# Mixed tiles of two experts in place of padded tiles, and a reordered convolution step, in a two-layer mixture of experts

## The chip, the cores and the metric

One core of a Trainium2 chip runs the program. The metric is the device time of one execution in microseconds; the median of three runs of the kernel before is 1354.1 (1354.05 to 1354.81). TensorE (PE) multiplies, VectorE (DVE) and ScalarE (ACT) work on tiles, GpSimd (POOL) issues the scatters, SyncE (SP) issues most of the other transfers. All times below are microseconds unless marked ns.

## What is computed

A causal convolution of seven taps over the sequence, with softmax taps for each head, and then two mixture-of-experts layers with one expert for each token. N is 14336 tokens of 192 values, 8 experts, 1024 hidden values. Cut to what matters:

```python
x = attn_out.reshape(N, 192)                # causal convolution, 7 taps for each of 8 heads
for layer in (0, 1):
    logits = x @ w_gate
    expert_idx = np.argmax(logits, axis=1)
    gate_w = softmax(logits)[np.arange(N), expert_idx]
    for e in range(8):
        mask = expert_idx == e
        h = np.maximum(x[mask] @ w1[e], 0.0)
        out[mask] = gate_w[mask, None] * (h @ w2[e])   # layer 1: times sigmoid(x @ w_output_gate)[mask, e] too
    x = out
```

## The kernel before

**Convolution steps.** Eight steps (`STEPS`) of 16 windows of 112 tokens. In each, PE convolves, DVE finds the largest value of each row and its power of two (`largest`), ACT and DVE scale the rows and split them into two float16 parts (`hi_ready`, then `low_rows`, lines 1029 and 1030), PE transposes them and computes the logits, DVE chooses an expert and a place (`step_choose`, `step_place`), and POOL writes the rows with 16 indirect DMAs (line 531) into the DRAM tensor `rows[0]`, in which each expert has a region of `CAP` rows. Beside it each step turns the weights of one expert of layer 0 into scaled float16 parts: SP loads them into `stage` (lines 332 to 337), DVE reduces them (`weights_max`, lines 1090 and 1092), POOL takes the maximum over partitions (`weight_maxima`, line 525), DVE makes the scale (`weights_scale`), ACT writes the high part and DVE the low part (`weights_lo`, lines 1105 and 1108), and SP stores the image and loads the next `stage` of that slot.

**Tables.** From the number of rows of each expert DVE makes a table (`table_counts`, `table_tiles`, `table_scales`): for each tile its first row and its expert. An expert with c rows gets ceil(c/256) tiles. Whatever the counts are, N/256 + E - 1 = 63 tiles a layer (`NT`) are enough, and 63 are always run; the last one or more can be empty. Rows behind the last row of an expert are filled by `store_pad` (line 350) with pad rows. In layer 1 the first 11 tiles (`EARLY`) are listed before the last rows of layer 0 are placed, and the rest later. The list is dealt out to even and odd tiles, so that each of the two weight slots keeps its expert over several tiles.

**Expert tiles.** A tile is 256 rows of one expert. `hidden` multiplies in four chunks (`NP`), each a PSUM bank of 2 x 256 columns: for each half of a chunk four matmuls of 256 columns, and `hidden_low` adds eight matmuls of 64 rows, which run in pairs in the two halves of the array. ACT takes the relu and its float16 high part (`relu_hi`, line 732), DVE the low part (`hidden_lo`, line 1214), and `contract` multiplies back, with 12 matmuls of 192 columns a chunk. `contract` of tile t for chunks 1 to 3 runs between the hidden chunks of tile t+1. In layer 0 the finished rows of each two tiles (a pair) are split, transposed, gated and scattered into `rows[1]`; tiles 4 to 35 of layer 0 also prepare the weights of layer 1.

**SP's queue in a tile** (`loads`, line 406): it waits until the hidden chunks of the tile before are done (`h_done`), reads from the table in SBUF the experts of tile g+1 and of tile g-1 (`expert`), which had the same slot, loads part 0 of the image (1 MB) only if they differ (line 404), and otherwise raises the semaphore itself; then `load_x` of tile g+2: one table read, two DMA transposes (lines 395 and 396) and the load of two values of each row (line 397); then it waits for `y_done` and does part 1 of the weights. `xT` has four buffers (`XS`), `wslot` has two.

What sets the order: each engine's queue is written out in program order, with semaphores between them; the first four tiles (`HEAD`), tiles 60 to 67 around the change of layer (`MID`) and the last (`TAIL`) are unrolled, the others are loops of four tiles.

Of the kernel before, what the change touches and what calls it, by code (L numbers as in the profile page):

```python
# [18 lines left out]
B, S, D = 4, 3584, 192  # L19
H, K = 8, 7  # L20
E, F = 8, 1024
N = B * S
P = 128
# [20 lines left out]
NT = N // T + E - 1  # L44
GT = 2 * NT
EARLY = 11
STAGES = ((0, 0, NT), (1, NT, EARLY), (1, NT + EARLY, NT - EARLY))
QUADS = NT // 4
PAIRS = (NT + 1) // 2
# [23 lines left out]
def build(nc, x, weight, wg0, w10, w20, wg1, wo1, w11, w21, out):  # L73
# [12 lines left out]
    with ctx:  # L86
# [10 lines left out]
        onesf = sb("onesf", [1, 1], f32)  # L97
# [8 lines left out]
        tidx = sb("tidx", [P, GT], f32)  # L106
# [58 lines left out]
        took = sb("took", [P, E], f32)  # L165
        start = sb("start", [P, 1], f32)
        ge = sb("ge", [P, NT, E], f32)
        gt = sb("gt", [P, NT, E], f32)
        te = sb("te", [P, NT], f32)
        tst = sb("tst", [P, NT], f32)  # L170
        tew = sb("tew", [P, NT], f32)
        tabD = sb("tabD", [P, GT], f32)
        tab = sb("tab", [P, 2, GT], i32)
# [65 lines left out]
        routed = sem("routed")  # L239
        token_ready = sem("token_ready")  # L240

        w_loaded = [[sem(f"w{part + 1}_loaded{i}") for i in range(2)] for part in range(2)]
        x_loaded = [sem(f"x_loaded{i}") for i in range(XS)]
        meta_loaded = [sem(f"meta_loaded{i}") for i in range(XS)]
        meta_out = sem("meta_out")
# [7 lines left out]
        FIRST = (NT // 2 + 1, NT // 2)  # L253
# [37 lines left out]

        def routes(g, s, l):
# [11 lines left out]
        HEAD, MID = range(0, 4), range(4 * QUADS, 4 * QUADS + 8)  # L304
        LOOPS = (((1, E + 1, True), (E + 1, QUADS, False)), ((QUADS + 2, GT // 4, False),))
        TAIL = range(GT // 4 * 4, GT)
        LAST = (GT - 1, (GT - 1) // 2, 1)
        assert NT % 4 == 3 and E + 1 < QUADS and STEPS == E and SPB == 2
# [14 lines left out]

        def pair_wins(p):

            return J if isinstance(p, int) and p == PAIRS - 1 else W2T
# [27 lines left out]
        def _(sp):  # L354
# [36 lines left out]

            def load_x(g, x, l):
                r0 = sp.value_load(tab[0:1, 1, bass.ds(g, 1)], min_val=0, max_val=ROWS - T)
                tile_rows = rows[l][bass.ds(r0, T), :]
                sp.dma_start_transpose(xT[:, x, 0:3, :], tile_rows.bitcast(f16)[:, 0:3 * P]).then_inc(x_loaded[x], 16)  # L395
                sp.dma_start_transpose(xT[:, x, 3:4, :], tile_rows.bitcast(f16)[:, DB:DB + P]).then_inc(x_loaded[x], 16)
                sp.dma_start(xmeta[:, x, :, :], tile_rows[:, D:RW].rearrange("(j p) c -> p j c", j=J)).then_inc(meta_loaded[x], 16)

            def expert(g):
                return sp.value_load(tab[0:1, 0, bass.ds(g, 1)], min_val=0, max_val=E - 1)  # L400

            def load_w_part(e, l, s, part):
                cols = (slice(0, W2H), slice(W2H, WCOL))[part]
                sp.dma_start(wslot[:, s, cols], images[l][bass.ds(e + l, 1), :, cols].rearrange("e p c -> (e p) c")).then_inc(w_loaded[part][s], 16)

            def loads(g, k, s, v, i, prep, l):
# [3 lines left out]
                ahead = layer_of(g + 1, l)  # L410

                def load_next(e, had, part):
                    if other:
                        load_w_part(e, ahead, 1 - s, part)
                    else:
                        with sp.If(e != had):
                            load_w_part(e, ahead, 1 - s, part)
                        with sp.Else():
                            sp.sem_inc(w_loaded[part][1 - s], 16)
# [20 lines left out]
            for e in range(E // 2):  # L440
                store_pad(sp, 0, e)
# [933 lines left out]
```

## Time and profile before

| | |
|---|---|
| median of 3 runs | 1354.1 us (1354.05 to 1354.81) |
| profiled execution | 1355.4 us, span 1353.8 us |
| instructions | 38270 |
| busy share | PE 90%, DVE 64%, ACT 47%, POOL 33% |
| mean granted clock of TensorE | 0.929 |
| tiles | 63 in each of two layers |

The page gives for each engine its busy time and share of the span, and the span in 40 slices of 33.8 us. The timeline gives single instructions with start and duration; in brackets stands how long the engine sat idle before an instruction and what released it. SPq is SP's queue: the duration of a DMA instruction there is the time for which it occupies the queue, not that of the transfer.

### The profile page before, as it was taken

What the parts mean: (1) busy time and instruction counts of PE and PEld (TensorE: products, weight loads), DVE (VectorE), ACT (ScalarE), POOL (GpSimd) and SP (SyncE); (2) the same over time, 40 slices, a digit from 0 to 9 for tenths busy, and PEclk for the clock granted to TensorE, in tenths of its full rate; (3) what the DMA queues carried; (4) which work ended last, traced back from release to release, by engine and by line L of the source; (5) the groups of instructions that cost most, each with busy time, mean ns of one, the idle gap of its engine ahead of it and who ended that gap; (6) DMA issues with size and microseconds to landing.
All of it is one profiled execution on the core that took longest, in us unless ns stands there. A gap on an engine that the chain in (4) does not pass through costs nothing.

```text
span 1353.8 us, 38270 instructions
## 1 busy us (share of the span) xinstructions
PE 1214.6 (90%) x13162; PEld 1092.6 (81%) x13162; DVE 869.7 (64%) x2322; ACT 638.7 (47%) x1126; POOL 451.5 (33%) x480
## 2 busy tenths in 40 slices
PE   3777683099999999999999999999999999999998
PEld 2666673088888888889999998888899999899997
DVE  3798887348999999997777777633433334333333
ACT  2676674135555555654444544433333333333342
POOL 1187777503333443332222222422222222222222
PEclk9666665599999999999999999999999999999999
DMA  8388856646876677553522246356442244262220
GB/s 231 90 261 272 254 191 193 212 99 160 228 191 159 160 195 206 140 150 84 130 50 55 54 102 147 74 148 166 109 110 61 56 103 106 57 164 59 55 52 17
DMA packets 237528, 181.20 MB, mean 134 GB/s; under 512 B 183263, under 2 KB 215675, under 8 KB 233890
## 3 DMA queue, kind: packets, MB, share of 16 engines
q1 hardware_dynamic: 209760, 114.76, 34.5%
q0 software_dynamic: 26096, 64.50, 15.6%
q10 hardware_dynamic: 1618, 1.26, 0.3%
q8 instruction: 29, 0.48, 0.2%
q14 instruction: 25, 0.20, 0.1%
HBM read 79.36 MB, written 70.80 MB: 111 GB/s over the span
## 4 chain that ended last, share of the span: by engine, by line
PE 56%; DVE 20%; issue 9%; DMA 7%; SPq 5%; ACT 2%; POOL 1%; DVEq 1%; ACTq 0%; POOLq 0%
PE bank L791 55%; DMA stage<-in_moe_w 5%; DVE hl L1214 2%; DVE wam L1090 2%; DVE split L1105 2%; DVE am L1021 1%; PE bank L796 1%; DVE xsl L1025 1%; DVE split L1108 1%; ACT rowt L642 1%; DMA wslot<-image 1%; POOL rows L531 1%; DVE rowab L1030 1%; DVE rowt L1030 1%; SPq L395 1%
## 5 line engine op out<-in xcount | busy, mean ns | idle before, releaser
L791 PE MATMUL bank<-xT,wslot 128*128 128x256 f16 (+1 forms) x5040 | 596.1, 273 | 40.3 <-DMA xT<-rows 33.7
L1214 DVE SCALAR_TENSOR_TENSOR hl<-bank,hh 128x512 f16<-128x512 f32 x504 | 347.6, 690 | 364.5 <-ACT hh L732 359.1
L791 PE MATMUL bank<-wslot,hh 128*128 128x192 f16 x4032 | 541.3, 246 | 0.0
L732 ACT ACTIVATE hh<-bank 128x512 f16<-128x512 f32 x504 | 300.6, 596 | 497.9 <-PE bank L791 488.9
L791 PEld LDWEIGHTS bank<-xT,wslot 128*128 128x128 f16 (+1 forms) x5040 | 420.3, 97 | 112.1 <-DMA xT<-rows 33.8
L791 PE MATMUL bank<-wslot,hl 128*128 128x192 f16 x2016 | 496.4, 246 | 0.0
L791 PEld LDWEIGHTS bank<-wslot,hh 128*128 128x128 f16 x4032 | 361.5, 98 | 28.4 <-issue 19.8
L611 POOL DMA_INDIRECT out_tokens<-y,idxt x126 | 122.8, 974 | 370.5 <-ACT y L744 323.6
L552 POOL DMA_INDIRECT rows<-rowt,idxp x126 | 133.2, 1057 | 338.7 <-PE bank L791 210.5
L791 PEld LDWEIGHTS bank<-wslot,hl 128*128 128x128 f16 x2016 | 197.4, 98 | 0.0
L642 ACT ACTIVATE rT<-bank 128x672 f16<-128x672 f16 (+1 forms) x127 | 97.9, 773 | 69.6 <-PE bank L796 69.5
L531 POOL DMA_INDIRECT rows<-rowab,idxa x96 | 111.8, 1165 | 55.4 <-issue 46.4
L791 PE MATMUL bank<-xw,band 128*112 128x192 f32 x256 | 74.9, 475 | 48.4 <-ACT conv L642 34.5
L744 ACT ACTIVATE y<-bank,tf 128x192 f32<-128x192 f32 x252 | 92.1, 416 | 52.6 <-PE bank L791 52.2
L791 PEld LDWEIGHTS bank<-xw,band 128*112 128x112 f32 x256 | 67.5, 274 | 51.7 <-ACT conv L642 34.0
L791 PEld LDWEIGHTS bank<-gs,rT 128*112 128x112 f16 (+1 forms) x762 | 50.4, 147 | 18.2 <-ACT rT L642 11.4
L791 PE MATMUL bank<-gs,rT 128*112 128x16 f16 (+1 forms) x762 | 57.3, 204 | 7.7 <-ACT rT L642 7.7
L1090 DVE TENSOR_REDUCE wam<-stage 128x1 f32<-128x2048 f32 x16 | 36.5, 2280 | 16.4 <-DMA stage<-in_moe_w 16.4
L796 PE MATMUL bank<-ident,rowab 112*128 112x112 f16 x288 | 30.1, 270 | 18.6 <-DVE rowab L1030 18.6
L531 POOL DMA_INDIRECT rows<-wslot,idxa x32 | 36.9, 1152 | 12.2 <-issue 9.1
L796 PEld LDWEIGHTS bank<-ident,rowab 112*128 112x128 f16 x288 | 24.0, 133 | 20.6 <-DVE rowab L1030 20.4
L1105 DVE SCALAR_TENSOR_TENSOR split<-stage,winv,split 128x2048 f16<-128x2048 f32 x16 | 37.5, 2343 | 2.1 <-ACT split L661 2.1
(145 smaller groups left out, 873.7 us busy)
## 6 DMA issues: line engine op xcount, KB each, us to landing
wslot<-image SPq DMA_DIRECT2D x20, 1024.0 KB, 5.6
wslot<-image SPq DMA_DIRECT2D x20, 768.0 KB, 4.7
image<-split POOLq DMA_DIRECT2D x18, 512.0 KB, 4.8
image<-split SPq DMA_DIRECT2D x8, 1024.0 KB, 4.4
image<-split POOLq DMA_DIRECT2D x9, 768.0 KB
xw<-in_x SPq DMA_DIRECT2D x4, 1536.0 KB, 11.5
stage<-in_moe_w SPq DMA_DIRECT2D x8, 768.0 KB, 10.2
image<-split SPq DMA_DIRECT2D x8, 768.0 KB, 6.2
```

The costliest lines, as they stand in the source:

```text
L531: nc.gpsimd.indirect_dma_start(rows[0][:, :], bass.IndirectOffsetOnAxis(idxa[0:WIN, n % SLOTS, w:w + 1], 0), rowa[n % SLOTS][0:WIN, w, :], ...
L552: nc.gpsimd.indirect_dma_start(rows[1][:, :], bass.IndirectOffsetOnAxis(idxp[:, v, j:j + 1], 0), rowt[:, v, j, :], None, bounds_check=ROWS ...
L611: nc.gpsimd.indirect_dma_start(out[:, :], bass.IndirectOffsetOnAxis(idxt[:, s, j:j + 1], 0), y[:, s, j, :], None, bounds_check=N - 1, oob_ ...
L642: return nc.scalar.activation(o, i, ACT.Copy)
L732: nc.scalar.activation(hh[:, c, :], bank[c][:, :], ACT.Relu).then_inc(hh_out, 1)
L744: last = nc.scalar.activation(y[:, s, j, :], bank[YB + s][:, j * D:(j + 1) * D], ACT.Identity, scale=tf[:, s, j:j + 1])
L791: return nc.tensor.matmul(o, a, b_, start=start, stop=stop, skip_group_check=True)
L796: last = nc.tensor.transpose(dst(c), src[:, c * P:(c + 1) * P], ident[0:src.shape[0], 0:src.shape[0]])
L1030: return V.tensor_tensor(row[:, :, D + DB:2 * D], scaled[:, :, 0:P], row[:, :, 0:P], ALU.subtract)
L1090: V.tensor_reduce(wam[:, slot, 0:1], stage[:, slot, 0:2 * F], AX.X, ALU.max, apply_absolute_value=True)
L1105: V.scalar_tensor_tensor(split[:, slot, 2 * F:W2H], stage[:, slot, 0:2 * F], winv[:, slot, 0:1], split[:, slot, 0:2 * F], ALU.mult, ALU.su ...
L1214: V.scalar_tensor_tensor(hl[:, c, :], bank[c][:, :], 0.0, hh[:, c, :], ALU.max, ALU.subtract).then_inc(hl_out, 1)
```

## The change

`NT` becomes 60 a layer: 49 tiles (`WHOLE`) of 256 rows of one expert as before, taken from the full tiles of each expert, counts rounded down, and then 11 mixed tiles (`MIXED`), each of two blocks of 128 rows with an expert and a first row of their own. 22 blocks a layer take what is left, counts rounded up to 128.

- In a mixed tile PE's `hidden` and `hidden_low` run with 128 columns for each block, with that block's weights: 80 matmuls in place of 40. `contract` has as many as before.
- There are four weight slots: two more, for the second blocks, in the memory of `split` and `stage`, which the steps have left by then.
- SP's `load_x` of a mixed tile is done once for each block, with 128 rows: four transposes in place of two. `loads` between mixed tiles reads four experts in place of two and has a branch for each slot; the second blocks' weights are first loaded two tiles ahead (`first`).
- The tables: a list of whole tiles and a list of blocks (`REST0`, made in tiles 0 and 1); in layer 1 three lists, of 11, 38 tiles and 22 blocks (made at `NT - 4` and `NT - 3`, `NT + 2` and `NT + 3`, `NT + 4` and `NT + 5`).
- Pads of layer 0 are stored by SP in tiles 0 to 3, behind each tile's loads, in place of four by SP and four by ACT before tile 0. SP waits for the scatters itself, without POOL's wait and `memset`.
- Convolution steps: DVE does the low rows ahead of both reductions of the weights; POOL takes the maximum between the two halves of the 16 scatters.
- 30 pairs of finished tiles in place of 32, the last of which was half.

The diff, cut to its core:

```diff
-NT = N // T + E - 1
+WHOLE = N // T - (E - 1)
+MIXED = (N // P + E - 1 - J * WHOLE + 1) // 2
+NT = WHOLE + MIXED
...
+        wslots = [wslot[:, 0, :], wslot[:, 1, :], split[:, 1, :], stage[:, 1, :].bitcast(f16)]
...
+        def mixed(g):
+            return isinstance(g, int) and g < GT and g % NT >= WHOLE
+        def weights_of(g, s, j):
+            return 2 + s if j and mixed(g) else s
...
+            def load_block(g, a, n, x, l, loaded, meta):
+                r0 = sp.value_load(tab[0:1, 1, a, bass.ds(g, 1)], min_val=0, max_val=ROWS - n)
+                here = slice(a * P, a * P + n)
+                tile_rows = rows[l][bass.ds(r0, n), :]
+                sp.dma_start_transpose(xT[:, x, 0:3, here], tile_rows.bitcast(f16)[:, 0:3 * P]).then_inc(loaded, 16)
+                sp.dma_start_transpose(xT[:, x, 3:4, here], tile_rows.bitcast(f16)[:, DB:DB + P]).then_inc(loaded, 16)
+                sp.dma_start(xmeta[:, x, a:a + n // P, :], tile_rows[:, D:RW].rearrange("(j p) c -> p j c", p=P)).then_inc(meta, 16)
             def load_x(g, x, l):
+                if mixed(g):
+                    load_block(g, 0, P, x, l, x_loaded[x], meta_loaded[x])
+                    load_block(g, 1, P, x, l, x2_loaded[x], meta2_loaded[x])
+                else:
+                    load_block(g, 0, T, x, l, x_loaded[x], meta_loaded[x])
...
                 if weights:
                     sp.sem_inc(store_turn, 1)
-                    e = expert(g + 1)
-                    had = None if other else expert(g - 1)
-                    load_next(e, had, 0)
+                    needs = [(expert(g + 1, 0), None if other else expert(g - 1, 0), 1 - s)]
+                    if again:
+                        needs.append((expert(g + 1, 1), expert(g - 1, 1), 3 - s))
+                    if first:
+                        needs.append((expert(g + 3, 1), None, 3 - s))
+                for need in needs:
+                    load_next(*need, 0)
...
-            sp.wait_ge(pads_ready, 1)
-            for e in range(E // 2):
-                store_pad(sp, 0, e)
...
-            sp.wait_ge(pads_stored, 16 * E)
-            sp.wait_ge(routed, 1)
+            for i in range(2 * SLOTS):
+                sp.wait_ge(scat_a[i], 8 * G * len(range(i // 2, STEPS, SLOTS)))
             load_x(0, 0, 0)
...
+            sp.wait_ge(pads_ready, 1)
             for g in HEAD:
                 one(loads, g)
+                for e in (2 * g, 2 * g + 1):
+                    store_pad(sp, 0, e)
...
                 if late(n, 1):
-                    scatter_step(n - 1)
+                    scatter_step(n - 1, 0)
                 weight_maxima(n, q)
+                if late(n, 1):
+                    scatter_step(n - 1, 1)
...
             def hidden(t, k, s, x, i, c):
...
                     for n, (w, xc) in enumerate(((0, 0), (0, 2), (1, 1), (2, 0))):
-                        last = mm(o, wcol(w), xT[:, x, xc, :], c == 0 and u == 0 and n == 0, n == 3)
+                        for j, (r0, rn) in enumerate(columns(t)):
+                            last = mm(bank[c][:, u * T + r0:u * T + r0 + rn], wslots[weights_of(t, s, j)][:, w * F + f0:w * F + f0 + P],
+                                      xT[:, x, xc, r0:r0 + rn], c == 0 and u == 0 and n == 0 and j == 0, n == 3)
...
             def step(n, b, q):
...
-                weights_max(q, stage_loaded[q], (b + 1) * 64, 0)
                 dve.wait_ge(hi_ready, n + 1)
                 row32 = rowa[n % SLOTS][0:WIN, :, :]
                 V.tensor_copy(row32[:, :, MI:MI + 1], ids[0:WIN, :].unsqueeze(2))
                 low_rows(xs[0:WIN, :, :], row32.bitcast(f16)).then_inc(lo_ready, 1)
+                weights_max(q, stage_loaded[q], (b + 1) * 64, 0)
                 weights_max(q, None, None, 1)
```

## Rows read from the trace of the kernel before

**Rows 1.** The page, busy time of each engine and its share.

```profile
PE 1214.6 (90%) x13162; PEld 1092.6 (81%) x13162; DVE 869.7 (64%) x2322; ACT 638.7 (47%) x1126; POOL 451.5 (33%) x480
```

**Rows 2.** Timeline of ACT, relu of a tile's first chunk: start, us, instruction.

```profile
706.00 0.60 ACT L732 ACTIVATE hh<-bank 128x512 f16<-128x512 f32 x1 [1.60 <-PE bank L791]
...
723.29 0.60 ACT L732 ACTIVATE hh<-bank 128x512 f16<-128x512 f32 x1 [1.59 <-PE bank L791]
...
1005.59 0.60 ACT L732 ACTIVATE hh<-bank 128x512 f16<-128x512 f32 x1 [1.60 <-PE bank L791]
...
1013.69 0.60 ACT L732 ACTIVATE hh<-bank 128x512 f16<-128x512 f32 x1 [1.59 <-PE bank L791]
```

**Rows 3.** Timeline of DVE over one convolution step.

```profile
189.12 2.29 DVE L1090 TENSOR_REDUCE wam<-stage 128x1 f32<-128x2048 f32 x1 [2.75 <-DMA stage<-in_moe_w]
...
194.73 1.74 DVE L1092 TENSOR_REDUCE wam<-stage 128x1 f32<-128x1536 f32 x1
...
198.73 1.81 DVE L1108 SCALAR_TENSOR_TENSOR split<-stage,winv,split 128x1536 f16<-128x1536 f32 x1
...
215.90 2.29 DVE L1090 TENSOR_REDUCE wam<-stage 128x1 f32<-128x2048 f32 x1 [3.66 <-DMA stage<-in_moe_w]
```

**Rows 4.** Timeline of SP's queue in the same step.

```profile
201.66 0.52 SPq L332 DMA_DIRECT2D stage<-in_moe_w  x1
```

**Rows 5.** Timeline of POOL: first scatter, and one batch of 16.

```profile
59.85 1.29 POOL L531 DMA_INDIRECT rows<-rowab,idxa  x1 [18.78 <-issue]
...
212.59 0.96 POOL L531 DMA_INDIRECT rows<-rowab,idxa  x1 [2.16 <-DVE idxa L1081]
...
235.64 0.32 POOL L525 PARTITION_ALL_REDUCE wmx<-wam  x1
237.42 0.96 POOL L531 DMA_INDIRECT rows<-rowab,idxa  x1 [1.45 <-DVE idxa L1081]
```

**Rows 6.** Timeline where the steps end and tile 0 begins.

```profile
259.05 0.94 POOL L531 DMA_INDIRECT rows<-rowab,idxa  x1 [0.30 <-issue]
...
264.12 1.33 SPq L395 DMA_TRANSPOSE xT<-rows  x1
...
268.42 5.82 PE L791 MATMUL bank<-xT,wslot 128*128 128x256 f16 x40 [33.69 <-DMA xT<-rows]
```

**Rows 7.** Waits of PE from 800 us on: in total, times, longest.

```profile
PE bank L791 <- DMA wslot<-image: 3.1, 3, 1.5
```

**Rows 8.** Timeline of PE in a routing tile of layer 0.

```profile
332.94 1.04 PE L791 MATMUL bank<-xT,wslot 128*128 128x256 f16 x8
333.81 0.33 PE L791 MATMUL bank<-wslot,hh 128*128 128x192 f16 x2
...
339.64 0.50 PE L796 MATMUL bank<-ident,rowt 128*128 128x128 f16 x6
339.98 1.74 PE L791 MATMUL bank<-xT,wslot 128*128 128x256 f16 x16
```

**Rows 9.** Timelines of PE and of SP's queue in layer 1.

```profile
1011.30 0.33 PE L791 MATMUL bank<-wslot,hh 128*128 128x192 f16 x2
...
1011.55 0.33 PE L791 MATMUL bank<-wslot,hh 128*128 128x192 f16 x2
...
996.83 0.35 SPq L404 DMA_DIRECT2D wslot<-image  x1
998.25 1.44 SPq L395 DMA_TRANSPOSE xT<-rows  x1
...
1014.01 1.26 SPq L395 DMA_TRANSPOSE xT<-rows  x1
1015.40 1.14 SPq L396 DMA_TRANSPOSE xT<-rows  x1
1016.75 0.42 SPq L397 DMA_DIRECT2D xmeta<-rows  x1
```

**Rows 10.** Weight loads of the tiles, from issue to landing.

```profile
DMA to landing us min/median/max: 4.2/5.3/7.8
```

More of the change, by code:

```diff
@@ L290, in in_order, with mixed_upto @@
                 one(body, g)
+        def mixed(g):
+            return isinstance(g, int) and g < GT and g % NT >= WHOLE
+        def mixed_upto(g, every):
+            return len([h for h in range(g % every, g + 1, every) if mixed(h)])
+        def weights_of(g, s, j):
+            return 2 + s if j and mixed(g) else s
         def routes(g, s, l):
@@ L410, in loads, with load_next @@
                 ahead = layer_of(g + 1, l)
-                def load_next(e, had, part):
-                    if other:
-                        load_w_part(e, ahead, 1 - s, part)
+                first = mixed(g + 3) and not mixed(g + 1)
+                again = mixed(g - 1) and mixed(g + 1)
+                def load_next(e, had, slot, part):
+                    if had is None:
+                        load_w_part(e, ahead, slot, part)
                     else:
                         with sp.If(e != had):
-                            load_w_part(e, ahead, 1 - s, part)
+                            load_w_part(e, ahead, slot, part)
                         with sp.Else():
-                            sp.sem_inc(w_loaded[part][1 - s], 16)
+                            sp.sem_inc(w_loaded[part][slot], 16)
                 weights = late(g, 1) and last + 1 < GT
-                e = had = None
+                needs = []
                 if late(g, 1):
@@ L468, in _ @@
                 sp.wait_ge(next_stored[part], (32, 16)[part] * (E + 1))
[L469 removed]
+            for g in range(NT - 1, NT + 4):
                 one(loads, g)
@@ L536, in _ @@
             steps(pool, step)
-            scatter_step(STEPS - 1)
-            for i in range(2 * SLOTS):
-                pool.wait_ge(scat_a[i], 8 * G * len(range(i // 2, STEPS, SLOTS)))
-            nc.gpsimd.memset(onesf[0:1, 0:1], 1.0).then_inc(routed, 1)
+            for half in range(2):
+                scatter_step(STEPS - 1, half)
             def paced(chunk):
@@ L556, in scatter_pair @@
             def scatter_pair(p, v):
-                for j in range(pair_wins(p)):
+                for j in range(W2T):
                     scatter_row(p, v, j)
@@ L870, in _, with columns @@
             step_ranks(STEPS - 1)
+            def columns(t):
+                return ((0, P), (P, P)) if mixed(t) else ((0, T),)
             def hidden_low(t, s, x):
```

305 lines of the change are left out of this document (173 added, 132 removed).

## Prediction, made before the changed kernel was built or run

> **What bounds the kernel now.** I read the page first. PE is busy 1214.6 of 1353.8 us, the next engine 869.7 [rows 1]; the slices show PE full from about 280 us on and thin before. So there are two kernels to look at: the convolution steps, in which PE waits, and 126 expert tiles, in which it rarely does. The timeline of ACT gives the pitch of the tiles: from one first `relu_hi` to the next 8.10 us in layer 1 (13.69 against 5.59), and 17.29 us for two tiles in the second half of layer 0, 8.65 each, where the routing of finished rows (transposes, logits, ranks) is added [rows 2]. Then the step: a DVE timeline shows one full step from 189.12 to 215.90, all of it work but the last 3.66 us, a wait for the weight load `stage` [rows 3].
>
> **The tiles that go.** Six tiles fewer (126 to 120) at 8.10 are -48.6. Three fewer with a routing share of 8.65 - 8.10 are -1.6 [rows 2]; the quads that prepare weights are unchanged in number.
>
> **The convolution steps.** `weights_max` of part 0 (L1090) stands ahead of the low rows in DVE's queue (L1029 and L1030), so these sit behind a load that lands last; they fill the 3.3 us between the end of L1090 (191.41) and L1092 at 194.73 [rows 3]. `hi_ready` is there by 212.24, when the wait begins (215.90 - 3.66), so the low rows would fit that hole. The loop load - maxima - `weights_lo` - next load then loses 3.3 us: the next load is issued at 201.66 [rows 4], lands 14.2 us later (215.90); from L1090 to the end of L1108 are 11.4 us (189.12 to 200.54), less 3.3 are 8.1, and 1.1 us go to the next issue (200.54 to 201.66): 23.4 instead of the 26.8 of this step [rows 3, 4]. What is late next is POOL: 16 scatters from 212.59 on, the maximum at 235.64 (0.32) and 0.3 to the next start make 23.65 us a step [rows 5]. Starting at 59.85 as now, the eighth batch can start no earlier than 59.85 + 7 x 23.65 = 225.4, against 237.42: -12.0 [rows 5]. The diff moves the maximum between the two halves of a batch, so DVE's `weights_scale` doesn't wait for the 16th scatter; that keeps this bound a pure POOL bound. The last batch then runs after most DVE work; four of its scatters were stretched by that work, which may give 1 us more. Ends: -5, if transfers (moved closer together) get slower by 1 us a step, and -15; I take -13. Behind it, the wait of POOL for the scatters and its `memset` go, which lay between the last scatter (259.05) and SP's first row load (264.12), 0.4 us of it handshake [rows 6]: -0.4.
>
> **What is moved, small.** Pads leave the stretch before tile 0, where they were hidden behind the scatters, and come into SP's queue behind the loads of tiles 0 to 3, two a tile, some 3 us a tile of SP's time with their table reads: SP is late by about 1 us for the weights of tile 3. DVE gets the second list of layer 0 (counts, tiles, scales; about 5 us) into tiles 0 and 1, ahead of a `hidden_lo`, for which PE has under 1 us of slack a tile. Together +2 (0 to 4). At the change of layer PE now waits 3.1 us for weights that SP issues among pads [rows 7]; in the new order the four tiles with pads (64 to 67) need no new expert, so -3 (-4 to 0). The DVE tables before tile `NT` stay as dear as they were.
>
> **PE's work in a mixed tile.** Columns are the same, but 40 matmuls of 256 become 80 of 128, each with a weight load. Eight matmuls of 256 columns take 0.87 us (332.94 to 333.81), 109 ns each; six transposes of 128 columns with six weight loads take 0.34 (339.64 to 339.98), 57 ns each [rows 8]. So 64 x 57 - 32 x 109 = +0.15 us a tile, and 22 tiles give +3.3; the 64-row halves could add as much again. The Trainium skill speaks against the change here: "TensorE: Matmul & The Clock Gate", section on sustained throughput, gives about 81 ns a matmul for a stream of weight load and matmul pairs at 128 columns. By it the 22 tiles would cost about +40. The rows above are such pairs and are faster, so I don't take it.
>
> **SP's queue in a mixed tile: the term that decides.** In a plain tile SP wakes when the hidden blocks of the tile before are done (1011.30), issues the first transpose at 1014.01 and the last load at 1016.75 + 0.43, 5.9 us in all of 8.1 [rows 9]. In it are two table reads of the expert and one of the row. From the weight load's end (997.18) to the next transpose (998.25) is 1.07 us for a row read and the end of a branch, so two expert reads, a branch and the waking take 1.7: 0.7 for a read, 0.25 for a branch. A transpose occupies the queue for 1.25 us with three column groups, 1.15 with one, the meta load 0.43, with some 0.15 between; `load_x` is 4.0 us [rows 9]. A mixed tile does `load_x` twice with 128 rows each, reads four experts, and has four branches. With unchanged issue times that is 4 x 0.7 + 4 x 0.25 + 2 x 4.0 + 0.4 = 12.2 us, with weight issues, against PE's 8.3 (layer 1) or 8.8 (layer 0). SP becomes the bound.
> How it reaches PE: part 0 of the weights for tile g+1 is issued in tile g, after all four expert reads, and lands 5.3 us later [rows 10]. Issued 3.3 us after waking it is ready at 8.6, just before the next tile (9.0 after waking); every us by which SP is late is then a wait of PE, if the expert of that slot changes. I worked out the lists from the reference with its inputs (rows per expert 1480, 1890, 1700, 2132, 1587, 1576, 2074, 1897 and 1487, 2411, 1284, 1648, 1883, 3227, 966, 1430): the first halves of the mixed tiles run 0,4,0,5,1,6,2,7,2,7,3 and 0,5,0,5,1,6,2,6,3,7,4 (every second entry shares a slot), so 8 of 11 tiles in each layer bring a new expert; the second halves are all expert 7. In the tiles without a change the lag is carried on, and paid at the next change.
> How long a transpose of 128 rows holds the queue, no row shows. Upper end: as now, 1.25 and 1.15, since a third of the columns saves only 0.10. Lower end: what any load costs (0.43, the meta load of the same rows) stays, and the remaining 0.82 and 0.72 halve with the rows: 0.84 and 0.79. I went through tiles 40 to 59 of both layers with these times (SP starts at the later of its own end and PE's hidden blocks; a tile starts at the later of PE's end and the landing): PE waits 17 + 23 = 40 us at about 0.85, 23 + 29 = 52 at 1.0, 33 + 39 = 72 at 1.25. With both at 0.6 (plain-load cost hardly there) it would be 20. I take the lower end, 0.8 to 0.85: bytes plainly don't matter, a fixed cost would have to be three times that of another load of the same rows, and rows are the one size that both transposes share. At 0.8 the walk gives 35; I take +37.
> The Trainium skill ("DMA: Bandwidth & Descriptors", the table of decode times) puts a small transpose at 631 cycles and a plain copy at 512 of the sequencer. The plain ones here take 0.35 to 0.43, in line with that; an estimate from the page for a small transpose is then about 0.45 us, so the 1.15 measured here would hold a part that grows with size, on the side of my choice.
>
> **Sum.** -48.6 - 1.6 - 13 - 0.4 + 2 - 3 + 3.3 + 37 = -24.3. The profiled execution is 1355.4 us (span 1353.8, 1.6 around it), so 1331.1; the median is 1.3 below it, so 1329.8, say 1330.
>
> **Rivals.**
> 1. *SP's issue cost is fixed, slower than before.* One mechanism: SP's queue in the mixed tiles at 12.2 us each. Without SP's term the sum is -61, so it decides from about 61 us of waits on, which is a transpose of some 1.1 us. At 1.2 to 1.25 it gives 67 to 72: 1360 to 1365. For it: three column groups cost hardly more than one. Against: the size of the cost beside a plain load.
> 2. *In between*, a transpose at about 1.0: 1345.
> 3. *SP hides it.* If 128 rows cost little more than a plain load (20 us of waits) or the weights arrive earlier than I have them: 1295 to 1312. For it: median landing is 5.3, the shortest 4.2 [rows 10].
> 4. *The steps don't get shorter*, since the loads just take longer when POOL's scatters and the loads come closer: +10 on the sum, 1340.
> 5. *A pair of weight load and matmul can't go below the pitch that the expert tiles show now.* Three pairs of 192 columns take 0.25 us (1011.30 to 1011.55), 82 ns each [rows 9]. If 128 columns took that too, 64 x 25 ns are 1.6 us a tile, 35 us over 22 tiles; SP's lag hides most of it, my walk gives +8 net, 1338. Against: the transposes at 57 ns [rows 8]. This is the mechanism that the page on TensorE, named above, would stand behind.
>
> **How the numbers follow.** Forecast 0.43, rival 1 0.24, rival 2 0.10, rival 3 0.13, rival 4 0.06, rival 5 0.04. The forecast's own range is 1320 to 1338. The range leaves out the fast end of rival 3 and the slow end of rival 1: 1298 to 1364. A measurement of this kernel can tell about 0.2% (2.7 us) from no change. Slower takes nearly all of rival 1, 0.23; the same takes its best end and the worst of rival 2, 0.05; faster 0.72.
>
> **What would show it.** Steps: no wait of L1090 for `stage`, POOL's batches 23.6 apart, the last scatter near 246 and tile 0, now at 268.42 [rows 6], near 255. Mixed tiles: L791's matmuls of 128 columns at 57 ns apart; SP's transposes near 0.85; PE idle before `xT` matmuls with `wslot<-image` as releaser, 35 to 40 us in all; mean pitch of the tiles 50 to 59 near 10.5 us. Wrong would be: transposes at 1.15 or more, POOL not back to back, or a pitch of 8.3 in the mixed tiles.

## The result, and the profile after

The changed kernel takes 1374.7 us (median of 4 runs, 1373.6 to 1375.7), beside 1354.5 for the kernel before on the same chip: a ratio of 1.0149, 95% interval 1.0131 to 1.0166. It is slower by 20 us (1.5%), clear of the noise, where 1330 was forecast and the range ended at 1364. The span of the profiled execution is 1374.1 us.

The page, busy time of each engine, and the chain that ended last by engine:

```profile
PE 1182.8 (86%) x13470; PEld 1069.3 (78%) x13470; DVE 847.1 (62%) x2277; ACT 615.7 (45%) x1083; POOL 436.1 (32%) x471
...
PE 42%; DVE 18%; SPq 14%; issue 14%; DMA 6%; ACT 3%; POOL 2%; DVEq 1%; POOLq 0%; ACTq 0%
```

PE has 32 us less to do than in [rows 1] and the kernel still takes longer; SP's queue stands in the chain with 14%, in the kernel before with 5%. The timeline of ACT, the first relu of a tile, as in [rows 2]; these are tiles 0, 10, 11, 48, 60, 108, 112, 113 and 119:

```profile
254.52 0.60 ACT L759 ACTIVATE hh<-bank 128x512 f16<-128x512 f32 x1 [32.55 <-PE bank L818]
...
343.12 0.60 ACT L759 ACTIVATE hh<-bank 128x512 f16<-128x512 f32 x1 [0.39 <-PE bank L818]
...
357.45 0.60 ACT L759 ACTIVATE hh<-bank 128x512 f16<-128x512 f32 x1 [0.84 <-PE bank L818]
...
685.82 0.60 ACT L759 ACTIVATE hh<-bank 128x512 f16<-128x512 f32 x1 [0.39 <-PE bank L818]
...
831.28 0.60 ACT L759 ACTIVATE hh<-bank 128x512 f16<-128x512 f32 x1 [0.39 <-PE bank L818]
...
1222.99 0.60 ACT L759 ACTIVATE hh<-bank 128x512 f16<-128x512 f32 x1 [1.59 <-PE bank L818]
...
1263.94 0.60 ACT L759 ACTIVATE hh<-bank 128x512 f16<-128x512 f32 x1 [3.62 <-PE bank L818]
...
1281.98 0.60 ACT L759 ACTIVATE hh<-bank 128x512 f16<-128x512 f32 x1 [11.47 <-PE bank L818]
...
1356.21 0.60 ACT L759 ACTIVATE hh<-bank 128x512 f16<-128x512 f32 x1 [4.92 <-PE bank L818]
```

Read as pitches, against the same relus of before:

| stretch | before | after | difference |
|---|---|---|---|
| start to first relu of tile 0 | 270.89 | 254.52 | -16.4 |
| tiles 0 to 9 | 88.3 | 88.6 | +0.3 |
| tile 10 | 8.80 | 14.32 | +5.5 |
| tiles 11 to 46 | 320.7 | 319.6 | -1.1 |
| rest of layer 0 (16 tiles; 13, of them 11 mixed) | 140.2 | 154.2 | +14.0 |
| the next 48 tiles | 395.4 | 391.7 | -3.7 |
| to the first relu of the last tile (14; 11) | 113.4 | 133.2 | +19.8 |
| behind it | 16.1 | 17.9 | +1.8 |

Three tiles fewer in each layer should have taken 24 to 26 us from rows five and seven of the table each. Instead a tile of the last stretch takes 12.1 us on the mean (133.2 / 11), one of them 18.0 (1263.94 to 1281.98). Against plain pitches (8.65 and 8.10) the tiles from 48 to 59 and from 108 to 118 cost 41.7 and 44.1 us more, 86 in all.

Not all of that is waiting. These two stretches and one of plain tiles (length, busy time of PE, PEld, DVE, ACT and POOL with counts, PE's granted clock, DMA share, GB/s):

```profile
685.82:831.28 145.46, 115.38 (x1674) 108.96 (x1670) 80.54 (x287) 51.67 (x96) 23.35 (x24) 0.92 0.59 155
1222.99:1356.21 133.22, 101.10 (x1388) 94.77 (x1384) 34.48 (x77) 34.33 (x66) 22.28 (x23) 0.91 0.54 149
1000.00:1100.00 100.00, 100.00 (x1089) 90.46 (x1088) 39.66 (x86) 39.23 (x76) 23.56 (x25) 1.00 0.32 74
```

PE stands idle for 30.1 and 32.1 us. It is also busy for longer than in as many plain tiles, 115.4 us against 12 x 8.65 and 101.1 against 11 x 8.10, by 11.6 and 12.0 us, at a granted clock of 0.92 and 0.91 where plain tiles have 1.00. So 62 of the 86 us are waits and 24 are slower work between them, of which PE's narrower matmuls are about 2 (0.09 us a tile, experiment 4).

### The profile page after: what moved, and what is told of

Same layout as the page of the kernel before. It is cut to its first block, busy times and chain, and to the rows that moved or that the text cites. A ratio compares the mean times of both kernels' runs of the same rounds, so it can differ in the third digit from the quotient of the medians.

```text
span 1374.1 us, 38468 instructions
## 1 busy us (share of the span) xinstructions
PE 1182.8 (86%) x13470; PEld 1069.3 (78%) x13470; DVE 847.1 (62%) x2277; ACT 615.7 (45%) x1083; POOL 436.1 (32%) x471
## 4 chain that ended last, share of the span: by engine, by line
PE 42%; DVE 18%; SPq 14%; issue 14%; DMA 6%; ACT 3%; POOL 2%; DVEq 1%; POOLq 0%; ACTq 0%
PE bank L818 42%; SPq L412 4%; SPq L413 4%; DMA stage<-in_moe_w 3%; DMA wslot<-image 3%; SPq L424 2%; DVE am L1059 2%; DVE hl L1279 2%; POOL rows L568 2%; SPq L414 2%; DVE split L1143 1%; SPq L409 1%; DVE xsl L1063 1%; DVE wam L1128 1%; DVE wam L1130 1%
## 5 line engine op out<-in xcount | busy, mean ns | idle before, releaser
L818 PE MATMUL bank<-xT,wslot 128*128 128x256 f16 (+3 forms) x4800 | 576.7, 266 | 90.6 <-DMA xT<-rows 35.8
L1279 DVE SCALAR_TENSOR_TENSOR hl<-bank,hh 128x512 f16<-128x512 f32 x480 | 330.9, 690 | 416.4 <-ACT hh L759 412.0
L818 PE MATMUL bank<-wslot,hh 128*128 128x192 f16 x3488 | 482.1, 247 | 10.2 <-SPq L445 3.5
L818 PE MATMUL bank<-wslot,hl 128*128 128x192 f16 x1744 | 431.2, 247 | 0.0
L818 PEld LDWEIGHTS bank<-wslot,hh 128*128 128x128 f16 x3488 | 310.6, 98 | 36.5 <-issue 22.7
L818 PEld LDWEIGHTS bank<-wslot,hl 128*128 128x128 f16 x1744 | 171.6, 98 | 0.2
L673 ACT ACTIVATE rT<-bank 128x672 f16<-128x672 f16 (+1 forms) x124 | 95.8, 777 | 50.2 <-PE bank L823 49.9
L818 PE MATMUL bank<-xT,stage 128*128 128x128 f16 (+1 forms) x480 | 64.0, 242 | 0.0
L818 PE MATMUL bank<-gs,rT 128*112 128x16 f16 (+1 forms) x744 | 51.9, 198 | 11.8 <-ACT rT L673 11.5
L818 PE MATMUL bank<-xT,split 128*128 128x128 f16 (+1 forms) x400 | 47.1, 223 | 0.0
L818 PEld LDWEIGHTS bank<-xT,stage 128*128 128x128 f16 (+1 forms) x480 | 46.8, 109 | 0.0
L1290 DVE COPY tid<-xmeta 128x2 f32<-128x2 f32 x120 | 24.5, 204 | 24.8 <-DMA xmeta<-rows 22.0
```

The lines of the kernel that those rows point to most:

```text
L673: return nc.scalar.activation(o, i, ACT.Copy)
L818: return nc.tensor.matmul(o, a, b_, start=start, stop=stop, skip_group_check=True)
L1279: V.scalar_tensor_tensor(hl[:, c, :], bank[c][:, :], 0.0, hh[:, c, :], ALU.max, ALU.subtract).then_inc(hl_out, 1)
```

## What SP's queue does in the mixed tiles

The timeline of SP's queue in layer 1: the first transposes of the mixed stretch, one whole tile, and the first transposes of tiles behind it:

```profile
1215.98 1.47 SPq L412 DMA_TRANSPOSE xT<-rows  x1
...
1275.90 1.22 SPq L412 DMA_TRANSPOSE xT<-rows  x1
1277.25 1.13 SPq L413 DMA_TRANSPOSE xT<-rows  x1
1278.58 0.43 SPq L414 DMA_DIRECT2D xmeta<-rows  x1
1279.73 1.21 SPq L412 DMA_TRANSPOSE xT<-rows  x1
1281.06 1.15 SPq L413 DMA_TRANSPOSE xT<-rows  x1
1282.39 0.44 SPq L414 DMA_DIRECT2D xmeta<-rows  x1
...
1288.40 1.23 SPq L412 DMA_TRANSPOSE xT<-rows  x1
...
1301.59 1.22 SPq L412 DMA_TRANSPOSE xT<-rows  x1
...
1338.15 1.22 SPq L412 DMA_TRANSPOSE xT<-rows  x1
```

A transpose of 128 rows holds the queue for 1.21 to 1.23 us with three column groups and 1.13 to 1.15 with one. With 256 rows it was 1.26 and 1.14 [rows 9]. So the hold hardly depends on the number of rows. `load_x` of a mixed tile is 7.6 us here (from its first table read at 1275.22 to 1282.83), and the whole round of SP's queue (1338.15 - 1215.98) / 10 = 12.2 us, the figure that the prediction had for this case; in layer 0 it is 12.3. That this round sets the pace, and not PE, the waits of SP's queue show, first for the kernel before in a stretch of 89 us of layer 1 (1200 to 1289):

```profile
SPq L436 <- PE bank L791: 17.1, 11, 1.8
SPq L426 <- PE bank L791: 4.1, 7, 0.6
```

and then, as its only wait, for the changed kernel in its mixed stretch of 133 us (1223 to 1356.2):

```profile
SPq L409 <- DVE tf L1292: 0.2, 1, 0.2
```

Before, the queue waited for PE in every tile; in the mixed tiles of layer 1 it never does, and PE waits for what the queue issues. The waits of PE, over the whole run (released by, us, times, longest):

```profile
PE bank L818 <- issue: 34.1, 17, 3.6
PE bank L818 <- DMA wslot<-image: 21.1, 5, 6.7
```

Before, the waits for weights came to 5.3 us. For "issue" the profile names no releaser; all 34.1 us of it lie in the two mixed stretches (19.3 and 14.8), and without SP's extra work (experiment 4) 6.3 are left. With them go 18.3 us for weights in these stretches and 5.0 us that end with a semaphore that SP raises itself (L445), 57 of the 62 us.

## The experiments

**1 and 2. The two halves of the change by themselves.** The steps of the changed kernel in the kernel before:

```diff
+                if late(n, 1):
+                    scatter_step(n - 1, 0)
                 weight_maxima(n, q)
+                if late(n, 1):
+                    scatter_step(n - 1, 1)
...
-                weights_max(q, stage_loaded[q], (b + 1) * 64, 0)
...
                 low_rows(xs[0:WIN, :, :], row32.bitcast(f16)).then_inc(lo_ready, 1)
+                weights_max(q, stage_loaded[q], (b + 1) * 64, 0)
                 weights_max(q, None, None, 1)
```

> The kernel before (63 tiles a layer, pads and tables as before) with the convolution steps alone reordered: low rows ahead of the weights' maxima on DVE, POOL's maximum between the two halves of a batch of scatters. In the changed kernel the first tile's relu begins at 254.5 us, against 270.9 before. If the reordered steps bring all of that, this kernel takes 1354.4 - 16 = 1338. If the steps bring only what POOL's bound allowed in my sum (12 to 13) and the rest comes from the pads and the handshake, 1341 to 1342. If the steps bring nothing (the loads get slower), 1354.

Measured: 1336.8, ratio 0.9865 (0.9838 to 0.9892). The first relu of tile 0 comes at 254.81, against 270.89. And the opposite, the changed kernel with the old order in the steps (the same diff, backwards):

> The changed kernel with the steps in the old order, so the tiles, tables and pads alone. If the two parts add up: 1374.7 + 13 to 16 = 1388 to 1391. If the stall of 5 us in tile 10 of the changed kernel's profile (14.3 us in place of 9.1, behind a slow load of stage) belongs to the earlier start, it is gone here and the time is 1383 to 1386.

Measured: 1387.4, ratio 1.0246 (1.0211 to 1.028); first relu at 266.54. So the steps give 17 us, as expected, and the tiles with their tables and pads cost 33. Tile 10 takes 14.9 us here too, so its stall doesn't come from the earlier start. In the front the parts don't add up: the others bring tile 0 forward by 4.4 us with the old steps, and by 0.3 with the new ones (254.81 to 254.52), which is less than the spread between kernels with the same front (252.2 to 255.3, the one run of experiment 10 apart). How the steps do it is in the changed kernel's timelines, DVE's first:

```profile
179.94 2.29 DVE L1128 TENSOR_REDUCE wam<-stage 128x1 f32<-128x2048 f32 x1
...
203.34 2.29 DVE L1128 TENSOR_REDUCE wam<-stage 128x1 f32<-128x2048 f32 x1 [0.28 <-DMA stage<-in_moe_w]
```

POOL's, the maxima of two steps and the last scatter:

```profile
143.55 0.33 POOL L561 PARTITION_ALL_REDUCE wmx<-wam  x1
...
166.96 0.32 POOL L561 PARTITION_ALL_REDUCE wmx<-wam  x1
...
244.61 0.94 POOL L568 DMA_INDIRECT rows<-rowab,idxa  x1 [0.30 <-issue]
```

The wait for `stage` is 0.28 us in place of 3.66 [rows 3], a step 23.4 us in place of 26.8, POOL works back to back (166.96 - 143.55 = 23.41), and its last scatter starts at 244.61 in place of 259.05 [rows 6].

**3 and 4. SP's transposes and reads taken away.** A mixed tile with one pair of transposes of 256 rows; that of the second block is left out, so its half of the tile is computed on other rows, and its semaphore is raised without it:

```diff
-                    load_block(g, 0, P, x, l, x_loaded[x], meta_loaded[x])
-                    load_block(g, 1, P, x, l, x2_loaded[x], meta2_loaded[x])
+                    load_block(g, 0, P, x, l, x_loaded[x], meta_loaded[x], T)
+                    load_block(g, 1, P, x, l, x2_loaded[x], meta2_loaded[x], 0)
```

> The changed kernel, but a mixed tile's xT is loaded by one pair of transposes of 256 rows from the first block's place; the second block's own transposes are left out (its table read and meta load stay), so the second halves of mixed tiles are computed on other rows. SP's queue in a mixed tile falls from about 12.2 us by 1.21 + 1.14 + 0.2 to about 9.8. If SP's queue is what bounds the mixed tiles, their waits fall from about 86 us to about 35 to 40 and the time from 1374.7 to 1325 to 1335. If PE's own work with 128 columns, or the landing of weights, is what costs, it stays above 1365.

Measured: 1311.1 (ratio 0.968, 0.9644 to 0.9715), 63.6 us less than the changed kernel, and below the 1325 to 1335 that were expected. Two transposes with what lies between them are 2.65 us of queue, 58 us over 22 tiles. Taking them away saves three quarters of the 86 us. In the two stretches PE's waits fall from 62 to 15.6 us and its busy time by 17, with the granted clock back at 0.98 in both. Then also without the second blocks' expert reads and branches:

```diff
-                    if again:
-                        needs.append((expert(g + 1, 1), expert(g - 1, 1), 3 - s))
...
+                    if again:
+                        sp.sem_inc(w_loaded[1][3 - s], 16)
```

> As e_onex, and SP doesn't read the experts of the second blocks either: their weights stay those loaded at first (with these inputs all of them are expert 7). SP's queue in a mixed tile is 0.7 + 0.6 us more than in a plain one, 7.5 to 8.3 us. SP theory: the pitch of the mixed tiles falls to 8.3 to 8.8 us in layer 1 and the time to 1354.4 - 16 - 49 - 2 + 3 to 10 = 1290 to 1300. Theory that pairs at 128 columns cost 82 ns: pitch 9.8 in layer 1, 1325.

Measured: 1303.5 (0.9624, 0.9591 to 0.9657), 3.5 us above the expected range and 22 under what pairs at 82 ns would have made. Mixed tiles 116 and 117 on ACT's timeline:

```profile
1257.85 0.60 ACT L766 ACTIVATE hh<-bank 128x512 f16<-128x512 f32 x1 [1.62 <-PE bank L825]
...
1266.04 0.60 ACT L766 ACTIVATE hh<-bank 128x512 f16<-128x512 f32 x1 [1.62 <-PE bank L825]
...
1274.24 0.60 ACT L766 ACTIVATE hh<-bank 128x512 f16<-128x512 f32 x1 [1.62 <-PE bank L825]
```

That is 8.19 us a tile, 0.09 over a plain one. What PE does in a mixed tile at full clock is nearly free; what costs is the queue that feeds it.

**5. The reads and branches alone taken away**, all four transposes kept (the second diff above, on the changed kernel):

> The changed kernel, but SP doesn't read the experts of the second blocks nor branch on them (these weights stay those loaded at first; with these inputs all are expert 7); the four transposes stay. SP's queue in a mixed tile falls by two reads and two branches, 1.9 us, to about 10.3. SP theory: pitch of the mixed tiles 10 to 11 us, PE waits 86 - 17 x 1.9 - the earlier issue = 35 to 50, time 1325 to 1342. If transposes alone cost, above 1365.

Measured: 1351.6 (0.997, 0.9956 to 0.9984), above the 1325 to 1342 that were expected. It is 23 us less than the changed kernel. The second blocks' reads stand only where the tiles on both sides are mixed (`again`), in 18 tiles and not 22, and they are shorter than the 1.9 us: in the changed kernel's trace four reads on SP take 2.27 us (1271.91 to 1274.17), 0.57 each, and a branch 0.17 (1271.59 to 1271.76). An estimate from these is 1.5 us a tile, 27 us in all. SP's first transposes are 10.7 us apart in layer 1 (1225.8 to 1311.7, eight tiles), 1.5 less than before, and the queue still waits only 1.5 us in a stretch of 120, so it stays the bound. In layer 0 its round fell by only 0.8 us, to 11.5; why, this run doesn't show.

**6. Is it when the weights are issued, or how long the queue is?** The first blocks' weights issued right behind their own two reads, that is two reads earlier (1.1 us at the 0.57 of experiment 5), same work:

```diff
                     needs = [(expert(g + 1, 0), None if other else expert(g - 1, 0), 1 - s)]
+                    load_next(*needs[0], 0)
```

> The changed kernel, with the load of the first blocks' weights issued after its own two table reads and not after four. SP's queue is as long as before; only part 0 comes 1.4 us earlier in each tile between mixed ones. If the landing of these weights after SP's lag is what PE waits for, 15 or 16 changes of expert each gain up to 1.4 us, but the queue's length stays the bound: -3 to -20, 1355 to 1372. If only the queue's length counts: within 2 us of 1374.7.

Measured: 1373.6 (1.0142, 1.0116 to 1.0169), 1 us under the changed kernel, within the intervals. The order inside the queue makes no difference that this run can tell (some 4 us would be needed); the queue again waited for almost nothing in the mixed stretches (0.5 and 0.0 us).

**7. Tile 10.** In the changed kernel's trace, SP's queue:

```profile
344.59 5.69 SPq L413 DMA_TRANSPOSE xT<-rows  x1
```

DVE's timeline:

```profile
348.35 1.75 DVE L1130 TENSOR_REDUCE wam<-stage 128x1 f32<-128x1536 f32 x1 [5.22 <-DMA stage<-in_moe_w]
```

And stretches of 10 us (length, busy time of PE, PEld, DVE, ACT and POOL with counts, PE's granted clock, DMA share, GB/s):

```profile
320.00:330.00 10.00, 9.72 (x119) 8.48 (x117) 9.42 (x24) 4.94 (x10) 4.57 (x5) 1.00 0.33 56
330.00:340.00 10.00, 9.83 (x114) 8.78 (x112) 9.21 (x29) 5.56 (x12) 4.59 (x5) 1.00 0.97 236
340.00:350.00 10.00, 8.51 (x104) 7.38 (x101) 4.78 (x6) 3.13 (x5) 0.56 (x1) 1.00 1.00 204
```

In the new list tile 10 is the first of the even tiles that has expert 1, so a set of weights (1.75 MB) is loaded from 333.45 on, while layer 1's weights for `stage` are under way: the DMA share is 0.97 and 1.00 over 20 us, DVE waits 5.22 us for `stage`, and one transpose holds SP's queue for 5.69. If that is the cause, another place for the change of expert takes it away. The two halves of layer 0's list are dealt out the other way round:

```diff
+                first, second = (n // 2, 0) if c0 == 0 else (0, (n + 1) // 2)
-                nc.gpsimd.iota(tidx[:, c0:c0 + n:2], [[1, (n + 1) // 2]], base=b0, channel_multiplier=0, allow_small_or_imprecise_dtypes=True)
-                nc.gpsimd.iota(tidx[:, c0 + 1:c0 + n:2], [[1, n // 2]], base=b0 + (n + 1) // 2, channel_multiplier=0, allow_small_or_imprecise_dtypes=True)
+                nc.gpsimd.iota(tidx[:, c0:c0 + n:2], [[1, (n + 1) // 2]], base=b0 + first, channel_multiplier=0, allow_small_or_imprecise_dtypes=True)
+                nc.gpsimd.iota(tidx[:, c0 + 1:c0 + n:2], [[1, n // 2]], base=b0 + second, channel_multiplier=0, allow_small_or_imprecise_dtypes=True)
```

> The changed kernel with the first list's halves swapped between even and odd tiles, so that expert 0 gives way to 1 at tile 11 or later and not at tile 10 (the same work). Tile 10 takes 14.3 to 15.4 us in all four profiles with 60 tiles, against 9.1; there, a weight change and the load and store of the prepared weights fill the DMA engines for 20 us. If the coincidence is the cause, no tile of 4 to 35 is above 10.5 us and the time is 1369 to 1371. If the list's position has nothing to do with it, tile 10 stays and the time is 1374.7.

Measured: 1370.6 (1.0129, 1.0106 to 1.0151), 4 us less, which the intervals alone would not tell from nothing; but tile 10 lasts 8.81 in place of 14.2 to 15.4 in every profile of 60 tiles with the other list, and no tile from 4 to 35 more than 9.41. The coincidence was the cause of this stall. It reached PE by way of `stage` and DVE: `oh`, which DVE makes behind the reduction that came 5.22 us late, is what PE waits for in tile 10, and the long transpose of SP released no wait of PE there:

```profile
352.27 0.19 PE L818 MATMUL bank<-oh,tri 128*128 128x32 f16 x1 [3.76 <-DVE oh L1084]
```

**8. Transposes of 128 rows without mixed tiles.** The kernel before, each tile's two transposes as four of half the rows:

```diff
-                sp.dma_start_transpose(xT[:, x, 0:3, :], tile_rows.bitcast(f16)[:, 0:3 * P]).then_inc(x_loaded[x], 16)
-                sp.dma_start_transpose(xT[:, x, 3:4, :], tile_rows.bitcast(f16)[:, DB:DB + P]).then_inc(x_loaded[x], 16)
+                for r in range(0, T, P):
+                    sp.dma_start_transpose(xT[:, x, 0:3, r:r + P], tile_rows[r:r + P, :].bitcast(f16)[:, 0:3 * P]).then_inc(x_loaded[x], 16)
+                    sp.dma_start_transpose(xT[:, x, 3:4, r:r + P], tile_rows[r:r + P, :].bitcast(f16)[:, DB:DB + P]).then_inc(x_loaded[x], 16)
```

> The kernel before (63 tiles a layer, no mixed tile, old steps), in which every tile's two transposes of 256 rows become four of 128 rows; weights, experts read and everything else stay. Fixed cost of a transpose: SP's queue needs 5.9 + 1.21 + 1.14 + 2 x 0.15 = 8.6 us a tile. In layer 1, where a tile lasts 8.10, it falls behind by 0.5 us a tile, paid at each change of expert: some 50 tiles x 0.5 = 25 us, 1375 to 1390; in layer 0 (pitch 8.53 to 9.2) nothing or little, and the transposes show 1.21 and 1.14. Cost that grows with the rows (my prediction, 0.80 to 0.85): 6.6 to 6.8 us a tile, 1354 to 1356. If it is instead something of the mixed tiles (weight loads beside them, memory reads) that holds transposes of 128 rows, they show under 1.0 here and the time stays within 3 us of before.

Measured: 1437.2, beside 1369.9 for the kernel before on that chip, ratio 1.0506 (1.0448 to 1.0564). SP's queue in layer 1:

```profile
1003.40 1.22 SPq L396 DMA_TRANSPOSE xT<-rows  x1
1004.75 1.14 SPq L397 DMA_TRANSPOSE xT<-rows  x1
1006.02 1.20 SPq L396 DMA_TRANSPOSE xT<-rows  x1
1007.35 1.15 SPq L397 DMA_TRANSPOSE xT<-rows  x1
1008.69 0.43 SPq L398 DMA_DIRECT2D xmeta<-rows  x1
...
1012.54 1.22 SPq L396 DMA_TRANSPOSE xT<-rows  x1
```

The same 1.20 to 1.22 and 1.14 to 1.15 us, in a kernel with no mixed tile and with few weight loads. That settles the size. The price was far above what I expected, 67 us where 21 to 36 had been worked out: from the first relu of tile 66 to that of tile 124 it takes 516.4 us (before 475.0), 8.90 a tile, where 8.6 was worked out; and tiles 0 to 65 take 608.3 (before 583.8, on another chip), with tiles of 12.8 to 13.3 us (11, 25, 41) where little or nothing was expected. From tile 66 to 124 SP's queue waited for PE for 104 us in the kernel before and for 1.0 us here; in the tiles ahead of that, 161 and 0.3 us. So it is the bound, and the 8.90 us are its own round, 0.3 more than was worked out, though no transpose there is long; where the 0.3 lie isn't shown.

**9 to 12. A version that takes the load off SP.** The first is experiment 9. For the mixed tiles the expert reads, the branches and the weight loads go to POOL's queue, between its scatters; SP keeps only the row loads. Where the expert stays, POOL loads 16 columns of the same image, so that the semaphore is raised by a transfer in either case:

```diff
+                    with pool.If(e != had):
+                        load_part(pool, e, l, slot, part, wp_loaded)
+                    with pool.Else():
+                        load_part(pool, e, l, slot, part, wp_loaded, 16)
```

> The changed kernel with the weight reads, branches and loads of tiles 47 to 58 (and 107 to 118) moved from SP's to POOL's queue; where the expert stays the same, POOL loads 16 columns of it in place of raising the semaphore. SP keeps the four transposes: 8.0 us of queue a mixed tile, about a tile of PE (8.19). SP theory: with SP just below the bound, the mixed tiles fall to 8.3 to 9.0 us; 1374.7 - 86 + 5 to 15 = 1295 to 1305, as the kernel with one pair of transposes. Rival, that two sets of transposes in one tile cost by their transfers (landing late) and not by SP's time: the mixed tiles stay above 10 us and the time above 1340.

Measured: 1320.0 (0.975, 0.9734 to 0.9767). 55 us under the changed kernel, 34 under the kernel before and 17 under the steps alone, but above the 1295 to 1305 that were expected. SP's row loads fit into a tile: SP's queue waits for PE again, 20.7 us in the stretch of layer 0. Six mixed tiles go at 8.19 and 8.62, one at 8.68 and one at 8.82, and the others at 9.2 to 11.6. PE's waits in the two stretches come to 11.0 and 8.0 us, and 13 of these 19 end with a load into `split` or `stage`, the slots of the second blocks; in layer 1 all such loads are the 16 columns. That POOL's loads come late there because they stand behind its scatters (0.96 us each) is my reading, not tested. With the other list of experiment 7 on top (experiment 10):

> The changed kernel with the mixed tiles' weight reads, branches and loads on POOL's queue (as in the run that gave 1320.0), and the halves of layer 0's first list dealt out the other way, so that no change of expert falls on tile 10 (as in the run that gave 1370.6, 4 less than the changed kernel with a tile 10 of 8.81). If the two parts are independent: 1320 - 4 to - 6 = 1314 to 1316, tile 10 at 8.8 in place of 14.6. If the stall moves with the new list to another tile beside POOL's stage loads, or the last mixed tiles of layer 0 get worse by their new neighbours: 1318 to 1322.

Measured, on the chip of experiment 8: 1345.2, beside 1369.9 for the kernel before, ratio 0.9811 (0.977 to 0.9851). Tile 10 went to 8.81, but tile 0 began 22 us later (275.77 against 253.70), and tiles 60 to 71 took 111.1 us against 99.7. Both might be the chip, so the two versions ran once more side by side (experiments 11 and 12):

> The changed kernel with the mixed tiles' weight reads, branches and loads on POOL's queue, a second time, now beside the version with the other list on one chip. 0.975 to 0.978 of the kernel before, tile 10 above 14.

> The same with the halves of layer 0's first list dealt out the other way, beside the version without that on one chip. If taking the change of expert off tile 10 is worth its 5 to 6 us here too, 4 to 6 us under the other version of this job (ratio about 0.972). If the 11.5 us that tiles 60 to 71 took more in the last job (111.1 from the first relu of tile 60 to that of tile 72, against 99.7) come with the list and not with the chip, it is 5 us or more above it.

Measured: 1322.5 (0.9777, 0.9741 to 0.9813) and 1321.8 (0.9743, 0.9713 to 0.9773): no difference that these runs can tell. Tiles 60 to 71 take 99.9 and 99.7 us with the two lists, so the late front and the slow layer change belonged to the other chip. Tile 10 gives 6.4 us (8.80 against 15.17), and the mixed tiles of layer 0, which get other neighbours, take 7.6 back (128.4 against 120.7 for tiles 48 to 59): the second case of what was expected of experiment 10. The 4 to 6 us that the list was expected to bring in experiment 12 are not seen: the medians are 0.7 us apart, and the intervals overlap.

## Why the prediction was wrong

**The step that failed** is the choice "I take the lower end, 0.8 to 0.85" for the hold of a transpose of 128 rows, and with it the +37 for the waits of the mixed tiles. Such a transpose takes 1.21 and 1.14 us, in the changed kernel and in experiment 8, and the mixed stretches cost 86 us. The mechanism, SP's queue as the bound, was right; its size was not. The argument, that a fixed cost would have to be three times that of another load of the same rows, was no evidence: it is three times that. The one pair of rows that bore on it, 1.25 for three column groups and 1.15 for one, said that size hardly counts, and I read from it only that bytes don't. Between two bounds with a sum of 40 and one of 72 us behind them, the nearer row was the transpose itself.

The decode-time table of the Trainium skill ("DMA: Bandwidth & Descriptors") has, in its column for the generations before, 631 cycles for a small transpose and 512 for a plain copy, from which came the estimate of about 0.45 us, on which I leaned too. Here no transpose of either size is below 1.13, and one of 128 rows holds the queue 2.7 to 2.8 times as long as the plain load beside it (1.14 and 1.21 against 0.43).

**Rival 1, point by point.** It is what happened, and was given 0.24. It had the queue at 12.2 us a mixed tile, and the trace has 12.2. In part that is luck: a table read takes 0.57 us and not 0.7, `load_x` of a mixed tile 7.6 and not 8.0, and 10 of the 88 transposes of mixed tiles hold the queue for 1.7 to 2.4 us, 8 us together over their usual time. What makes them long isn't shown; the DMA share is 0.59 and 0.54 in the two stretches. Rival 1 had 67 to 72 us of waits and a time of 1360 to 1365; the mixed stretches cost 86. A queue that never waits makes each of these tiles as long as its own round: 11 x (12.2 - 8.65) + 11 x (12.2 - 8.10) = 84 us over plain tiles. The walk came to 72 since it let the first tiles of each stretch start with a free SP. It had no slower clock of PE either, but where SP's queue sets the pace, slower work of PE takes the place of waiting: 62 + 24 us.

**The other terms.**
- Steps: -13 predicted, -16.1 found up to the first relu of tile 0 (experiment 1; -17 in the whole time), by the mechanism that was named: 23.4 us a step, POOL as the bound. The last scatter came 14.4 us earlier (246 was predicted, 244.6 found), and tile 0 another 1.7 closer behind it, which I had not counted. The handshake: -0.4 predicted; it can't be told, since kernels with the same front differ by up to 3 us there.
- Head and second list: +2 predicted, +0.3 found over tiles 0 to 9; the other profiles of 60 tiles with this list have 87.4 to 89.6 us there, so this is good to about 1 us.
- Layer change: -3 predicted, -3.7 found over 48 tiles.
- PE's 128 columns: +0.15 us a tile predicted, +0.09 found (8.19 against 8.10, experiment 4). The timeline of PE in a mixed tile, and two stretches around the wait ahead of it:

```profile
1233.46 0.22 PE L818 MATMUL bank<-xT,wslot 128*128 128x128 f16 x1 [3.61 <-issue]
1233.52 0.22 PE L818 MATMUL bank<-xT,stage 128*128 128x128 f16 x1
1233.58 0.22 PE L818 MATMUL bank<-xT,wslot 128*128 128x128 f16 x1
1233.63 0.22 PE L818 MATMUL bank<-xT,stage 128*128 128x128 f16 x1
1233.69 0.22 PE L818 MATMUL bank<-xT,wslot 128*128 128x128 f16 x1
...
1234.15 0.31 PE L818 MATMUL bank<-xT,wslot 128*128 128x128 f16 x1
1234.26 0.31 PE L818 MATMUL bank<-xT,stage 128*128 128x128 f16 x1
...
1223.00:1233.40 10.40, 6.85 (x76) 6.26 (x72) 3.15 (x7) 3.11 (x6) 2.82 (x3) 1.00 0.91 218
1233.90:1234.90 1.00, 1.00 (x12) 0.83 (x8) 0.00 (x0) 0.00 (x0) 0.00 (x0) 0.50 0.54 106
```

  Pairs of weight load and matmul start 55 to 60 ns apart, so rival 5 falls; so does, for this kernel, the 81 ns of the Trainium skill ("TensorE: Matmul & The Clock Gate", section "Back-to-back issue gap", on sustained throughput). The last two matmuls are 110 ns apart: the granted clock fell behind the wait of 3.6 us before 1233.46, from 1.00 to 0.50, the 1.2 GHz level.
- Not foreseen: tile 10, +5.5. The new list moved a change of expert beside the loads of layer 1's weights. I had worked out the lists for the mixed tiles and not asked where the changes of the plain ones fall.
- Rival 4 (steps not shorter) fell with experiment 1; rivals 2 (a transpose at 1.0) and 3 (SP hides it) fell with the 1.21 and the 12.2 us.

So the sum, with the sizes that were found: -50.2 for the tiles that go, +86 for the mixed stretches (PE's columns are in it), +5.5 for tile 10, -16.4 for the front, +0.3, -3.7, -1.1 and +1.8 from the table are +22.2, against +20.3 found. The kernel before had a wait of its own in what is now the mixed stretch (its tile 61 lasts 10.60 in place of 8.77, 1.8 us), which the plain pitch leaves out.

## What to carry to other kernels

When a tile is cut into smaller loads, count the instructions of the queue that issues them, at their present price, before the engine that computes: here PE had 32 us less to do and lost more by waiting for a queue that went from 5.9 to 12.2 us in a tile of 8. Where a row shows that one dimension of a transfer hardly changes its issue time, take the cost as fixed until a row shows otherwise. And when a list of work is reordered, look where its rare, dear entries (a new expert) fall beside transfers that already fill the DMA engines.

## What the runs showed of the hardware

- A DMA transpose holds SP's queue for 1.25 and 1.15 us at 256 rows (384 and 128 columns) and 1.21 and 1.14 at 128 rows, a plain load of two values of each row 0.43.
- Single transposes held the queue far longer: 5.69 us once, at a DMA share of 1.00, and 1.7 to 2.4 us in 10 of the 88 of mixed tiles, at 0.59 and 0.54.
- Reading an entry of a table in SBUF takes 0.57 us of SP's queue (four in 2.27 us), of which the load itself is 0.27.
- In stretches where PE stood idle for 30.1 of 145.5 and 32.1 of 133.2 us, its granted clock was 0.92 and 0.91 on the mean; in plain tiles without waits it was 1.00.
- One chip took 1369.9 us for the kernel before, where the others took 1354 to 1356. In the version run on both, tile 0 began 21 us later there and tiles 60 to 71 took 11.5 us more, while the plain tiles of layer 1 had 8.1 us on the mean on both.
